# Routing the first four of nine token tiles ahead of the other five, between attention and a mixture of experts

## The reference

```python
x = attention(q, k, v)                      # q (2, 8, 1152, 64) pooled by 2: 576 rows per batch and head
x = x.transpose(0, 2, 1, 3).reshape(1152, 512)

logits = x @ w_gate                         # 1152 x 8
e_idx = argmax(logits, axis=1)              # one expert per token
gate_w = softmax(logits)[e_idx]
eom = sigmoid(x @ w_output_gate)[e_idx]
for e in range(8):                          # w1[e] 512 x 1024, w2[e] 1024 x 512
    out[e_idx == e] = gate_w * eom * (relu(x[e_idx == e] @ w1[e]) @ w2[e])

h = out @ w_in                              # 512 x 2048
result = (h * tanh(log1p(exp(h)))) @ w_out  # 2048 x 512
```

## Time and profile before

| | |
|---|---|
| median of 3 runs | 728.31 us (727.35 to 730.36) |
| the profiled execution | 724.18 us, of it span 722.6 us |
| mean granted TensorE clock | 0.983 |
| busy share of the span | TensorE 93%, VectorE 70%, ScalarE 56%, GpSimd 12% |
| attention ends, first expert matmul starts | 292.35 us, 316.07 us |

### The profile page before, as it was taken

One profiled execution on the slowest core, in us unless ns is written; L12 is line 12 of the kernel. 1 busy time (PEld: TensorE's weight loads), 2 busy tenths in 40 slices (PEclk: granted clock), 3 DMA queues, 4 the chain that ended last, 5 costly groups with the idle time before them and its releaser, 6 DMA issues.

```text
span 722.6 us, 14642 instructions
## 1 busy us (share of the span) xinstructions
PE 674.6 (93%) x5121; PEld 596.0 (82%) x5122; DVE 506.7 (70%) x1145; ACT 403.0 (56%) x801; POOL 89.5 (12%) x123
## 2 busy tenths in 40 slices
PE   4899999999999999779999999993799999999997
PEld 3788888888888888578998999992698999899895
DVE  4677677767777675646656556656799978777874
ACT  4656675666666676125555555665566555455543
POOL 2304040404032100220000000005100000000000
PEclk9999999999999999899999999996999999999999
DMA  8578979797967400469961993103100010001001
GB/s 200 128 222 213 297 186 251 174 263 165 260 158 187 114 3 1 161 238 401 392 237 44 319 350 145 44 29 104 57 1 0 1 44 1 0 1 44 0 1 44
DMA packets 92384, 98.98 MB, mean 137 GB/s; under 512 B 41584, under 2 KB 65136, under 8 KB 91824
## 3 DMA queue, kind: packets, MB, share of 16 engines
q1 hardware_dynamic: 87984, 86.81, 40.8%
q0 software_dynamic: 2480, 8.13, 3.2%
q10 hardware_dynamic: 1872, 3.41, 1.5%
HBM read 62.16 MB, written 19.66 MB: 113 GB/s over the span
## 4 chain that ended last, share of the span: by engine, by line
PE 87%; DVE 4%; another core or an unknown queue 2%; issue 2%; ACT 2%; DMA 1%; POOL 0%; SPq 0%; ACTq 0%; DVEq 0%; POOLq 0%
PE score_banks L926 13%; PE score_banks L963 13%; PE turn L759 11%; PE pvT L740 11%; PE score_banks L940 10%; PE score_banks L716 5%; PE score_banks L717 4%; PE score_banks L980 4%; PE turn L980 4%; PE pvT L980 4%; PE turn L688 1%; PE turn L913 1%; PE turn L766 1%; DVE nmax_part L1176 1%
## 5 line engine op out<-in xcount | busy, mean ns | idle before, releaser
L759 PE MATMUL turn<-ident,prob 128*128 128x128 f32 x648 | 110.2, 279 | 4.3 <-DVE probT L1240 3.0
L1176 DVE TENSOR_REDUCE nmax_part<-score_banks 128x1 f32<-128x768 f32 x72 | 68.9, 958 | 59.4 <-PE score_banks L717 45.9
L926 PEld LDWEIGHTS score_banks<-xsT,w_slot 128*128 128x128 f32 x832 | 96.0, 195 | 7.6 <-issue 6.7
L926 PE MATMUL score_banks<-xsT,w_slot 128*128 x832 | 96.9, 278 | 5.7 <-ACT xsT L1074 4.1
L759 PEld LDWEIGHTS turn<-ident,prob 128*128 128x128 f32 x648 | 76.5, 140 | 26.1 <-issue 14.2
L1009 ACT ACTIVATE prob<-score_banks,nmax 128x1152 f32<-128x1152 f32 x72 | 87.6, 1217 | 3.9 <-DVE nmax L1186 3.9
L740 PE MATMUL pvT<-probT,v_sb 128*64 128x128 f32 (+1 forms) x1404 | 85.9, 269 | 0.0
L1350 DVE TENSOR_TENSOR w_lo<-w_slot,w_hi 128x512 fp32r<-128x512 f32 x104 | 71.8, 693 | 19.1 <-ACT w_hi L1089 19.0
L1016 ACT ACTIVATE probT<-turn 128x384 f32<-128x384 f32 x72 | 35.4, 491 | 87.7 <-PE turn L759 87.7
L716 PE MATMUL score_banks<-kT,qT 128*128 128x384 f32 x192 | 80.2, 418 | 3.8 <-DVE qT L1205 3.5
L740 PEld LDWEIGHTS pvT<-probT,v_sb 128*64 128x64 f32 x1404 | 69.5, 137 | 11.8 <-issue 11.8
(11 more groups left out here) (204 smaller groups left out, 1350.1 us busy)
## 6 DMA issues: line engine op xcount, KB each, us to landing
w_slot<-moe_w SPq DMA_DIRECT2D x16, 2048.0 KB, 13.3
slots_dram<-zeros SPq DMA_DIRECT2D x8, 1408.0 KB, 11.2
raw_k<-k SPq DMA_DIRECT2D x16, 288.0 KB, 5.5
v_sb<-v SPq DMA_DIRECT2D x16, 288.0 KB, 4.1
raw_q<-q SPq DMA_DIRECT2D x16, 256.0 KB, 3.9
w_in_sb<-moe_w_in SPq DMA_DIRECT2D x1, 4096.0 KB, 13.2
w_out_sb<-moe_w_out SPq DMA_DIRECT2D x1, 4096.0 KB, 14.8
kT<-k_hi SPq DMA_DIRECT2D x14, 288.0 KB, 4.5
```

The source lines that it names most:

```text
L759: last = pe.transpose(bank[:, j * P:(j + 1) * P], prob[:, s % 2, c * KC + j * P:c * KC + (j + 1) * P], ident[:, :])
L926: last = pe.matmul(h1_bank[f % 4][:, 0:P], w1_e[:, d, f * P:(f + 1) * P], xsT[:, d, bass.ds((t % XS_RING) * P, P)], start=(d == 0), stop=( ...
L1176: dve.tensor_reduce(nmax_part[:, s, 0:1], scores[s % 2][:, lo:lo + 2, 0:KC], AX.XY, ALU.max, negate=True).then_inc(max_part, 1)
```

## The change

The nine token tiles are routed in two batches: tiles 0 to 3 (`EARLY = 4`) and tiles 4 to 8.

- TensorE turns the last columns of tiles 0 to 3 at the end of step 15 of the last pass, makes their logits at the end of step 16, turns these in step 17, and makes their ranks after the last `pv`. ScalarE copies between.
- VectorE chooses for them ahead of the last two group ends, and picks gates, computes slots and gains and makes one-hots for them after the last x write. Then it does the same for the late batch.
- ScalarE scales the four early tiles (`scale_early`), VectorE the five late ones.
- GpSimd scatters a tile of the early batch when that batch's slots and the tile's scaling are there.
- TensorE places early tile 0 ahead of the late ranks and the rest after them.
- The banks of the early logits and ranks are those that attention's scores have left. `logitT` moves to the space of `q_pair`.

```diff
+    EARLY = 4
-        turn_tiles = [range(0, 4), range(4, 6), range(6, TPH)]
+        turn_tiles = [range(0, EARLY), range(EARLY, 6), range(6, TPH)]
+        batches = [range(0, EARLY), range(EARLY, TPH)]
...
 SyncE
-            sp.wait_ge(logits_turned, 1)
+            sp.wait_ge(logits_turned, 2)
             load_w1(2, 2)
...
 GpSimd
-            pool.wait_ge(slots_ready, 1)
             for i in range(TPH):
-                pool.wait_ge(x_scaled, i + 1)
+                if i < EARLY:
+                    pool.wait_ge(slots_ready, 1)
+                    pool.wait_ge(early_x_scaled, i + 1)
+                else:
+                    pool.wait_ge(slots_ready, 2)
+                    pool.wait_ge(x_scaled, i - EARLY + 1)
                 pool.indirect_dma_start(slots_dram, ...)
...
 TensorE, in the steps of the last pass
                     turn_p(s, 1).then_inc(p_turned, 1)
+                    if final and s == SB - 1:
+                        pe.wait_ge(logits_copied, 1)
+                        pe.transpose(score_banks[:, 3, 0:P], early_logitT[:, :], ident[:, :]).then_inc(logits_turned, 1)
...
+                    if final and s == SB - 3:
+                        pe.wait_ge(x_written, NIT * GB - 3)
+                        turn_last_d(0)
+                    if final and s == SB - 2:
+                        pe.wait_ge(wg_landed, 32)
+                        pe.wait_ge(last_d_copied, 1)
+                        early_logits().then_inc(logits_done, 1)
                 if final:
                     ...
                     turn_o(GB - 2, it, turn[0]).then_inc(p_turned, 1)
+                    early_ranks()
                     pe.wait_ge(x_written, NIT * GB - 2)
-                    for n in range(2):
-                        turn_last_d(n)
+                    turn_last_d(1)
...
+            def early_logits():
+                for d in range(DT):
+                    for t in range(EARLY):
+                        last = pe.matmul(early_logit_bank[t * GROUP:t * GROUP + 2 * NE, 0:P], w_both[:, d, :],
+                                         xrT[:, d, t * P:(t + 1) * P], start=(d == 0), stop=(d == DT - 1))
+            def late_logits(d):      # three matmuls of 256 columns: tiles 4, 5 / 6, 7 / 8 twice
+            def early_ranks():       # after chosen_ready 1 and gates_exp 2: one triangular, three of ones
+            def late_ranks():        # after chosen_ready 2: one triangular, nine of ones (early tiles too)
...
 TensorE, after the last pass
-            for d in range(DT - 1):
-                logits_of(d)
+            for d in range(2):
+                late_logits(d)
             pe.wait_ge(x_written, NIT * GB)
             turn_last_d(2)
+            late_logits(2)
             pe.wait_ge(last_d_copied, 3)
-            logits_of(DT - 1).then_inc(logits_done, 1)
+            late_logits(DT - 1).then_inc(logits_done, 1)
             pe.wait_ge(logits_copied, 2)
             ...                      # two turns in place of three
+            place_first(0)
+            late_ranks()
+            for t in range(1, TPH):
+                last = place_first(t)
...
 ScalarE, after the last pass
+            gates(0)
+            copy_last_d(1)
+            act.wait_ge(early_gain_ready, 1)
+            scale_early(0)
+            copy_last_d(2)
+            scale_early(1)
+            act.wait_ge(logits_done, 2)
+            act.activation(logitT[0:3 * GROUP, :, :], logit_bank..., ACT.Copy).then_inc(logits_copied, 1)
+            for t in range(2, EARLY):
+                scale_early(t)
+            gates(1)
...
 VectorE, after the last step
+                    choose(0)
+                    sign_slots(0)
                     for k in (GB - 2, GB - 1):
                         end_group(k, it)
                     ...              # the last x writes
+            pick(0)
+            gain_inverse(0)
+            dve.reciprocal(gain[:, 0:EARLY], gain_inv[:, 0:EARLY]).then_inc(early_gain_ready, 1)
+            place(0)
+            for t in range(EARLY):
+                mark(t)
+            choose(1)
+            sign_slots(1)
+            pick(1)
+            place(1)
+            gain_inverse(1)
+            then(dve.reciprocal(gain[:, EARLY:], gain_inv[:, EARLY:]))
+            for t in range(EARLY, TPH):
+                dve.tensor_scalar(x_tok[:, t, :], x_tok[:, t, :], gain[:, t:t + 1], None, ALU.mult).then_inc(x_scaled, 1)
+                mark(t)
```

More of the change, by code:

```diff
@@ L853, in turn_last_d @@
                 last.then_inc(last_d_turned, 1)
[L855 to L861, removed]
+            def early_logits():
[3 more added lines that the diff above has]
+                                         xrT[:, d, t * P:(t + 1) * P], start=(d == 0), stop=(d == DT - 1))
+                return last
@@ new lines, in late_logits @@
+            def late_logits(d):
+                for part in range(3):
+                    t = EARLY + 2 * part
+                    if t + 1 < TPH:
+                        rows_of = xrT[:, d, t * P:(t + 2) * P].rearrange("p (a n) -> p a n", a=2)
+                    else:
+                        rows_of = xrT[:, d, t * P:(t + 1) * P].unsqueeze(1).broadcast_to([P, 2, P])
+                    last = pe.matmul(logit_bank[part * GROUP:part * GROUP + 2 * NE, 0:2 * P].rearrange("p (a n) -> p a n", a=2),
+                                     w_both[:, d, :], rows_of, start=(d == 0), stop=(d == DT - 1))
+                return last
@@ new lines, in early_ranks @@
+            def early_ranks():
+                pe.wait_ge(chosen_ready, 1)
+                pe.wait_ge(gates_exp, 2)
+                pe.matmul(ranks[0], tri[:, :], chosen[:, 0:EARLY, :], start=True, stop=False)
+                for i in range(EARLY - 1):
+                    last = pe.matmul(ranks[0][:, i + 1:, :], ones[:, :],
+                                     chosen[:, i:i + 1, :].broadcast_to([P, EARLY - 1 - i, NE]),
+                                     start=False, stop=(i == EARLY - 2))
+                last.then_inc(ranks_done, 1)
@@ new lines, in late_ranks @@
+            def late_ranks():
+                pe.wait_ge(chosen_ready, 2)
+                pe.matmul(ranks[1], tri[:, :], chosen[:, EARLY:, :], start=True, stop=False)
+                for i in range(TPH):
+                    first = max(i + 1, EARLY)
+                    last = pe.matmul(ranks[1][:, first - EARLY:, :], ones[:, :],
+                                     chosen[:, i:i + 1, :].broadcast_to([P, TPH + 1 - first, NE]),
+                                     start=False, stop=(i == TPH - 1))
+                last.then_inc(ranks_done, 1)
@@ L863, in _, with place_first @@
+            def place_first(t):
+                pe.wait_ge(onehot_ready, t + 1)
+                if t < EARLY:
+                    pe.wait_ge(early_x_scaled, t + 1)
+                else:
+                    pe.wait_ge(x_scaled, t - EARLY + 1)
+                for d in range(DT):
+                    last = pe.matmul(first_fill[:, d, :], x_tok[:, t, d * P:(d + 1) * P], onehot[:, t, :],
+                                     start=(t == 0), stop=(t == TPH - 1))
+                return last
             pe.wait_ge(ident_ready, 2)
@@ new lines, in sign_slots, with pick @@
+            def sign_slots(n):
+                tiles, count = slice(batches[n].start, batches[n].stop), len(batches[n])
+                then(dve.tensor_tensor(signed[:, tiles, :], chosen[:, tiles, :], spread(slot_sign[:, :], count, NE), ALU.mult))
+            def pick(n):
+                tiles, count = slice(batches[n].start, batches[n].stop), len(batches[n])
+                dve.wait_ge(gates_exp, 2 * n + 2)
+                then(dve.tensor_tensor(both[:, tiles, :, :], both[:, tiles, :, :],
+                                       chosen[:, tiles, :].unsqueeze(2).broadcast_to([P, count, 2, NE]), ALU.mult))
+                then(dve.tensor_reduce(picked[:, tiles, :], both[:, tiles, :, :], AX.X, ALU.add))
+                then(dve.tensor_reduce(gate_sum[:, tiles], gate_exp[:, tiles, :], AX.X, ALU.add))
@@ new lines, in place @@
+            def place(n):
+                tiles = slice(batches[n].start, batches[n].stop)
+                dve.wait_ge(ranks_done, n + 1)
+                then(dve.tensor_tensor(slot[:, tiles, :], ranks[n][:, 0:len(batches[n]), :], signed[:, tiles, :], ALU.mult))
+                then(dve.tensor_reduce(slot_part[:, tiles], slot[:, tiles, :], AX.X, ALU.add))
+                then(dve.tensor_tensor(slot_f[:, tiles], slot_part[:, tiles], picked[:, tiles, 0], ALU.add))
+                dve.tensor_copy(slot_idx[:, tiles], slot_f[:, tiles]).then_inc(slots_ready, 1)
@@ L1314, in _ @@
[L1314 to L1317 removed]
+            def for_tiles(t):
+                return spread(t, ROW_TILES, NE)
+            pick(0)
[4 more added lines that the diff above has]
+                mark(t)
```

145 lines of the change are left out of this document (71 added, 74 removed).

## The result

The changed kernel took 721.84 us (median of 8 runs, 719.57 to 725.8) beside 728.07 for the kernel before (8 runs, 724.72 to 730.62): a ratio of 0.992, 95% interval 0.9891 to 0.995. That is 0.8% faster, and 721.8 was the forecast. The profiled execution took 722.0 us (span 720.4).

The account below looks back on a forecast made before the run. TensorE bounds the kernel almost everywhere except the routing between attention and experts, so the gain is an earlier first expert matmul: 724.18 - 6.5 = 717.7 profiled, 721.8 with the 4.13 difference kept; forecast 720.3 to 723.3, range 717.5 to 726.3.

Parts of the forecast that it names:

- the 0.8 us: After the last x write: ScalarE's first early scaling, queued ahead, makes the last copy of x 0.8 us late.
- rival 1: TensorE's clock stays up and the 3.2 us lag goes: up to 10.8 us gained, 717.5 to 720, chance 0.14.
- the price of 2.2 us: VectorE's late chain: cost if scatters slow ten operations; by the port rule gain 4.3, time 724.0; 0.2 was taken.
- 0.72 us for each late tile: Late routing: five scale and one-hot tiles at the nine tiles' old pace, last one-hot at 303.8 for 306.98.
- the half clock: Placing at 1.2 GHz: matmuls 0.166 us apart, 1.33 per tile; five or six tiles cost 0.44 more, ending at 308.4.
- the second path of the sum: First expert matmul at half clock as before, released by placing: 309.3, 6.8 us earlier.
- released by placing: First expert matmul comes 0.9 us after the last placing matmul: 306.9 at full clock, 309.3 at half clock.
- the 3.2 us: Unexplained lag from last placing matmul to ScalarE's copy of expert rows; tied to scatters or only the profiled execution's, both open.
- 6.5 us between 6.8 and 5.9: Gain taken between half clock with the lag kept (6.8) and full clock with the lag absent from timed runs (5.9).
- rival 2: Copy of expert rows goes on starting with the scatters' landing: gain 5.4 us, time 722.9, chance 0.15.
- a landing at 309.9: Last five scatters end issuing at 308.1 and land 1.75 us later, at 309.9 for 315.15 before.
- two paths that were not the path: Sum's placing-released paths: half clock as before, 6.8 us earlier; full clock without the 3.2 us lag, 5.9.

Follow-up runs that it names:

- the last three versions of the changed kernel: Changed kernel with three scatters behind placing (0.9955 of before), with ScalarE's last copy of x first (0.9947), and with both plus VectorE's bank mark before the tables (0.9953).
- the last version: Changed kernel with ScalarE's last copy of x first, last three scatters behind the placing, VectorE's bank mark ahead of the tables: 719.85 us, 0.9953 of before.

## Why the prediction was right

The time was right, the way there only in part, and so the time in part by luck.

*Right, nearly to the row* (aligned times):

| | forecast | measured |
|---|---|---|
| last x write, later than before | 1.0 | 0.93 |
| last copy of x starts | 295.1 | 295.08 |
| late choice starts | 297.0 | 297.26 |
| gains done | 300.3 | 300.57 |
| tables done | 308.0 | 307.59 |
| first scatter | 296.4 | 296.2 |
| last scatter's issue ends | 308.1 | 308.45 |
| placing ends, at full clock | 306.0 | 306.28 |

So ScalarE's queue did cost the 0.8 us, and the first half of rival 1 came true: the clock didn't fall. The scatters beside the late chain cost VectorE nothing that the rows show: the five late scalings stay at 0.48 us. So the price of 2.2 us by the port rule of the Trainium skill ("Advanced Engine Details and Errata", VectorE Performance Modes), weighed in the prediction, isn't borne out.

*Two terms off.* The forecast kept 0.72 us for each late tile. It took 0.59 (one-hots at 304.62 and 305.21); the diff also dropped VectorE's wait between scaling and one-hot, which is the likely reason. Last one-hot 303.37 for 303.8. And the half clock was misread: 23 records in 4.92 us are 0.214 us apart and 1.71 a tile, not 0.166 and 1.33; the first two marks of the kernel before lie 1.71 us apart. Four such tiles fill the 6.8 us at half clock, so by this estimate the second path of the sum is worth about 5.9 us and not 6.8. Neither showed in the result: TensorE was not waiting for the last one-hots, and the clock didn't fall.

*The step that failed* is "released by placing". The prediction made the first expert matmul the last placing plus 0.9, took the 3.2 us as possibly the profile's own, and chose 6.5 us between 6.8 and 5.9. What released it was neither the placing nor, quite, rival 2's landing (in after the copy starts 2.5 us ahead of the landing), but TensorE's count, held until 1.0 to 1.8 us behind the last scatter's issue. The placing came 5.7 us earlier and the scatters' issue 4.9; with 0.8 less behind it (1.0 us in after, 1.8 before) that makes the 5.68. The change paid because the scatters start 5.7 us earlier, by distance 20.64 for 26.38: with the scatters put back the gain is gone, and 2.3 us of faster placing alone bought nothing. Rival 2 gave 5.4 and 722.9, closer in mechanism than the forecast was. It also counted on a landing at 309.9; it came at 312.0, and the prediction had not counted on the fuller DMA beside it.

*What was given back.* The half clock in the first expert tile doubled from 3.41 to 6.83 us, which the prediction did not have; that it makes up the 1.36 us is argued from the clock alone. In the profile TensorE has nothing to do from 308.12 to 312.23, as it had before from 311.97 to 316.07.

*Where luck came in.* Up to the end of that expert line the two profiles, aligned, differ by 5.68 - 1.36 = 4.3 us, over the whole span by 4.0. The timed runs differ by 6.2, with an interval of 3.6 to 7.9 that holds both. The changed kernel with one unread turn, whose profile has the same distances, came out at 0.9939 of before, 4.4 us. So the mechanism accounts for some 4 us; that the median fell on 6.2, next to the 6.5 taken between two paths that were not the path, is in part chance.

*What stays open.* How much the change alone is worth on a chip that doesn't hold the counts: the unedited changed kernel wasn't run there. With three scatters behind in both kernels, the first expert matmul comes 4.9 us earlier with the change (32.37 for 37.28). Whether it is the chip: no kernel was profiled on both kinds, and that the kernel before is 4.6 to 5.7 us faster on the two that don't hold speaks for it; the held copy explains 3.2 of this, the rest is open. And what in a scatter holds a count, GpSimd's issuing or the transfers: the copy comes 1.0 to 1.9 us behind the last issue, and from 0 to 2.5 us ahead of the landing.

## What to carry to other kernels

When an engine starts several microseconds after the record that should release it, don't call the gap an artefact: find what ends at the same time on the other queues, and put a small waiting operation on an idle engine to see when each count arrives. Speeding up the chain that seems to end last is worth nothing while something else holds its count (2.3 us of faster placing moved the copy by 0.1), and a cover that goes lays the next one bare: here the scatters' hold, then TensorE's start into the expert loop, which hangs on VectorE's bounds. When the profile names a releaser, look at the waiting engine's sequencer before moving it: the bank mark was named and was not it. Times of the same kernel differed by up to 0.8% between chips, so kernels that are compared belong on the same one.

## What the hardware showed that was not expected

- On two chips TensorE's counts were held for up to 6.9 us past the matmul's record while GpSimd's indirect scatters ran, then came in a burst, three tiles' marks within 0.3 us. ScalarE's counts in the same stretch were on time. On two other chips, in four profiled kernels (in three of them the last three scatters were moved), the counts came within 0.05 us of the records, beside running scatters too.
- The kernel before takes 728.55 and 728.71 us on the former two, 723.95 and 722.99 on the latter.
- TensorE's start into the expert loop takes 3.0 to 3.2 us from the bounds that it reads, 1.10 to 1.36 of it the two reads. In the last three versions of the changed kernel 1.73 to 2.00 us of it lie bare behind the placing; where the copy comes late, or the bounds come 3.5 us before the placing ends (kernel before), it is hidden.
- The granted clock was 0.50 for 6.83 us in the first expert tile after 4.1 us without a matmul in after, 0.50 for 3.4 us after the same 4.1 us in the kernel before, 0.50 for 3.4 us after 2.0 us without one in the version with the copy moved, and 1.00 in the last version, after 1.73 us (stretches, as above):

```profile
307.10:314.00 6.90, 6.86 (x61) 6.87 (x62) 3.78 (x11) 3.60 (x11) 2.08 (x3) 1.00 0.51 176
```
